# Hash matmuls of two token halves in the two column halves of the array, key bits written with their factor, first load in two parts

## The chip, the cores and the metric

One Trainium2 chip, one of its cores. The metric is the device time of one launch in microseconds (us), the median of the timed runs. The engines are TensorE (PE), VectorE (DVE), ScalarE (ACT), GpSimd (POOL) and the DMA queue fed by SyncE (SP).

## What is computed

Three stages follow each other: hashed attention over 2 x 8 heads, a token and channel mixer, and a mixture of four attention experts. The change is in the first. Cut to what matters there:

```python
q_bits = (np.einsum('bhsd,dk->bhsk', q, proj) > 0)      # 6 bits for each query
k_bits = (np.einsum('bhsd,dk->bhsk', k, proj) > 0)      # 6 bits for each key
mask   = bucket(q_bits)[..., None] == bucket(k_bits)[..., None, :]
scores = np.where(mask, q @ k.T / sqrt(64), -1e9)
attn   = softmax(scores);  out = attn @ v
```

Sequence 768, head dimension 64, 16 heads. Everything is float32 in and out.

## The kernel before

**Tiling.** One head is one turn of the body. Queries come in six tiles of 128 rows, keys in two column halves of 384 (`HALF`). `psS` has two slots of two banks each, in which score tiles and hashes take turns; `psT` takes transposed probabilities, `psO` the products with the values.

**How the mask gets into the scores.** `scores` (L286, L287) adds two products for each key half. Rows 0 to 63 of the operands hold the split parts of queries and keys; rows 64 to 127 of `q_hb` and `k_lb` hold bits. For each of the six bits there is a row for "is one" and a row for "is not one", the key rows multiplied by 2^31 (`BIG`), so that a pair that agrees in all bits gets one common large offset, which the row maximum takes off again.

**The hash.** `hash_both(h+1)` (L259) runs in the body of head h: two fp32 matmuls, one for each token half, with the 128 x 128 projection `pj`, whose blocks give the key hashes on partitions 0 to 37 and the query hashes on 64 to 101. The result fills both banks of the slot that scores(h, 2) needs next. `query_bits` (L464) and `key_bits` (L475) on DVE then read 64 partitions x 768 of it. The query bits go straight to `q_hb`; the key bits go to a bf16 tile `bits`, which POOL multiplies by 2^31 into `k_lb` (`scale_key_bits`, L579).

**Order.** Each engine's order is written out by hand in its `head` function; semaphores join them. On DVE it runs: row_max(h,0) (L440), scale_and_bias (L449, L450), add_halves(h-2,1) (L493), turn(h-1,4) (L457), query_bits(h+1), key_bits(h+1), reciprocals(h-1) (L483, L485), row_max(h,1). On PE: scores(h,0), transposes (L300), hash_both(h+1), value_products(h-1,0) (L317), which waits for add_halves(h-2,1), scores(h,1), transposes, scores(h,2), fold (L328), transposes, scores(h,3), value_products(h-1,1), and so on. scores(h,3) waits for exp(h,1) (L377 on ACT). On POOL: scale_q (L548), round_k (L556), split_k (L563), split_q (L571), scale_key_bits (L579), normalise (L590) twice. ACT's round_q (L402) follows exp(h,0) and releases split_q.

**The start.** A first block builds constants while SP issues the projection and the whole of head 0's q and k (768 KB); a second block issues head 1's and holds the heads. The prologue of head 0 runs on every engine: hash, 12 matmuls on the identity (L63), round and copy q, round k on ACT (L411), split q on POOL, both bit operations and then the k split (L509) on DVE, and L579 on POOL, before scores(0,0).

Of the kernel before, what the change touches and what calls it, by code (L numbers as in the profile page):

```python
# [25 lines left out]
P = 128  # L26
# [6 lines left out]
NB = 6  # L33
NBP = 32 + NB
BIG = 2.0 ** 31
SCALE = 1.0 / D ** 0.5
R = 32
FF = 4 * C
# [75 lines left out]
def hashed_attention(nc, load_mixer, load_mlp_weights, mixer_in, u_rep, qk_2, v_n, proj_2, con, psS, psT, psO, X):  # L114
# [12 lines left out]
    with ExitStack() as ctx:  # L127
# [12 lines left out]
        q8 = sb("q8", [D, S])  # L140
        bits = sb("bits", [P, S], BF16)
        probs = [sb(f"probs{n}", [P, S]) for n in range(3)]
# [7 lines left out]
        rinv = sb("rinv", [P, 2, QT])  # L150
        q_comp = sb("q_comp", [P, 1])
        k_comp = sb("k_comp", [P, 1])
        pj = sb("pj", [P, P])
# [4 lines left out]
        cleared = sem("cleared")  # L158
        hashed = sem("hashed")
        q_bits_made = sem("q_bits_made")  # L160
# [8 lines left out]
        k_split = sem("k_split")  # L169
        kmask_ready = sem("kmask_ready")  # L170
        scores_ready = sem("scores_ready")
# [46 lines left out]
        def start_loads(sp):  # L218
            sp.dma_start(pj[:], proj_2).then_inc(proj_in, 16)
            load_qk(sp, 0, 0)  # L220

        build_constants(nc, ctx, con, start_loads)
        with nc.Block() as block:
            @block.sync
            def _(sp):
                load_qk(sp, 1, 1)
                load_v(sp, 0, 0)

                def next_loads(h, p):
                    sp.wait_ge(kmask_ready, h + 1)  # L230
                    sp.wait_ge(q_copied, h + 1)
                    if not low_bound(h, 1):
# [12 lines left out]
                load_v(sp, LAST - 1, 1)  # L245
                load_mixer(sp)
                load_mlp_weights(sp)

            @block.tensor
            def _(pe):  # L250
                def hash_both(h, p):

                    if not exists(h):
                        return
                    pe.wait_ge(raw_in[p], half_count(h, p))
                    if low_bound(h, 2):
                        pe.wait_ge(exp_done, 6 * (h - 1))
                    for c in range(2):
                        last = nc.tensor.matmul(psS[:, hash_slot(p), c, 0:HALF], pj[:],  # L259
                                                raw[p][:, c * HALF:(c + 1) * HALF], start=True, stop=True)  # L260
                    last.then_inc(hashed, 1)

                def scores(h, p, j):
                    if not exists(h):
                        return
                    slot = score_slot(p, j)
                    if j == 0:
                        pe.wait_ge(kmask_ready, h + 1)
                        pe.wait_ge(q_copied, h + 1)
                        pe.wait_ge(q_bits_made, h + 1)  # L270
                        if low_bound(h, 1):
                            pe.wait_ge(exp_done, 6 * h - 1)
                        else:
                            pe.wait_ge(first_k_split, 1)
                    elif j == 1:
                        pe.wait_ge(exp_done, 6 * h + 1)
                    elif j == 2:
                        if below(h, LAST - 1):
                            pe.wait_ge(q_bits_made, h + 2)
                            pe.wait_ge(k_bits_made, h + 2)  # L280
# [91 lines left out]
            def _(act):  # L372
# [23 lines left out]
                def round_q(h, p):  # L396
                    if not exists(h):
                        return
                    act.wait_ge(raw_in[p], half_count(h, p))
# [9 lines left out]
                def prologue():  # L409
                    round_q(0, 0)  # L410
                    nc.scalar.activation(k_hh[0][:], raw[0][:, S:2 * S], ACT.Copy).then_inc(first_k_rounded, 1)  # L411
                    copy_q(0, 0)

# [21 lines left out]
            def _(dve):  # L435
# [23 lines left out]

                def query_bits(h, p):  # L460
                    if not exists(h):
                        return
                    dve.wait_ge(hashed, h + 1)
                    nc.vector.tensor_scalar(q_hb[p][D:P, :].rearrange("p (c n) -> p c n", c=2),  # L464
                                            psS[D:P, hash_slot(p), :, 0:HALF], 0.0, q_comp[D:P, :],
                                            ALU.is_gt, ALU.subtract).then_inc(q_bits_made, 1)

                def key_bits(h, p):

                    if not exists(h):  # L470
                        return
                    dve.wait_ge(hashed, h + 1)
                    if low_bound(h, 1):
                        dve.wait_ge(kmask_ready, h)
                    nc.vector.tensor_scalar(bits[D:P, :].rearrange("p (c n) -> p c n", c=2),  # L475
                                            psS[0:D, hash_slot(p), :, 0:HALF], 0.0, k_comp[0:D, :],
                                            ALU.is_gt, ALU.subtract).then_inc(k_bits_made, 1)

# [18 lines left out]
                def prologue():  # L497

                    nc.vector.memset(q_comp[:], 0.0)
                    nc.vector.memset(k_comp[:], 0.0).then_inc(cleared, 1)  # L500
                    dve.wait_ge(cleared, 1)
                    nc.vector.memset(q_comp[D + 32:D + 32 + NB, :], 1.0)
                    nc.vector.memset(k_comp[0:NB, :], 1.0).then_inc(cleared, 1)
                    dve.wait_ge(cleared, 2)
# [35 lines left out]
            def _(pool):  # L540

                def scale_q(h, p):
                    if not exists(h):
                        return
                    pool.wait_ge(raw_in[p], half_count(h, p))
                    if low_bound(h, 1):
# [26 lines left out]

                def scale_key_bits(h, p):
                    if not exists(h):
                        return
# [17 lines left out]
                def prologue():  # L594
                    scale_q(0, 0)
                    split_q(0, 0)
                    scale_key_bits(0, 0)

                def head(h, p):
# [3 lines left out]
                    split_q(h + 1, 1 - p)  # L603
                    scale_key_bits(h + 1, 1 - p)
                    normalise(h - 2, p, 1)
# [1067 lines left out]
```

## Time and profile before

| | |
|---|---|
| timed runs, us | 732.81 median of 3 (732.45 to 734.55) |
| the profiled execution's own time, us | 733.43 |
| its span, us | 731.5 |
| busy in the span | PE 694.2 (95%), DVE 384.7 (53%), ACT 390.5 (53%), POOL 298.2 (41%) |
| granted TensorE clock, mean | 0.995 |
| masked heads | from the start to 277 us |

The time outside of the span is 1.9 us. A timeline row gives start, duration, engine, line, operation and tiles (out<-in), the shape, the count merged into the row, and in brackets the idle time of that engine before it with what ended it. Busy shares are averages over three stages; what the change is worth is read from the rows of the first 277 us.

### The profile page before, as it was taken

What the parts mean: (1) busy time and instruction counts of PE and PEld (TensorE: products, weight loads), DVE (VectorE), ACT (ScalarE), POOL (GpSimd) and SP (SyncE); (2) the same over time, 40 slices, a digit from 0 to 9 for tenths busy, and PEclk for the clock granted to TensorE, in tenths of its full rate; (3) what the DMA queues carried; (4) which work ended last, traced back from release to release, by engine and by line L of the source; (5) the groups of instructions that cost most, each with busy time, mean ns of one, the idle gap of its engine ahead of it and who ended that gap; (6) DMA issues with size and microseconds to landing.
All of it is one profiled execution on the core that took longest, in us unless ns stands there. A gap on an engine that the chain in (4) does not pass through costs nothing. (4 is left out here: it accounts for less than half of the span.)

```text
span 731.5 us, 11874 instructions
## 1 busy us (share of the span) xinstructions
PE 694.2 (95%) x3792; PEld 544.9 (74%) x3792; DVE 384.7 (53%) x827; ACT 390.5 (53%) x795; POOL 298.2 (41%) x260
## 2 busy tenths in 40 slices
PE   5899999999999998999999999999999989999986
PEld 3667666667666756788888888888888978788864
DVE  4888888888888846111112111211112757886571
ACT  3777776777777745333333333333333656676662
POOL 6655656545555111444544454345443012331210
PEclk9999999999999999999999999999999999999999
DMA  4112211112210594200000000000000000001102
GB/s 154 44 55 83 80 54 54 54 54 67 93 55 11 102 321 122 58 0 0 0 0 0 0 0 0 0 0 0 0 0 14 17 1 0 2 0 44 44 1 87
DMA packets 27548, 30.58 MB, mean 42 GB/s; under 512 B 11136, under 2 KB 21504, under 8 KB 27520
## 3 DMA queue, kind: packets, MB, share of 16 engines
q1 hardware_dynamic: 27520, 30.23, 13.3%
q8 instruction: 15, 0.25, 0.1%
q14 instruction: 13, 0.11, 0.0%
HBM read 27.07 MB, written 3.15 MB: 41 GB/s over the span
## 5 line engine op out<-in xcount | busy, mean ns | idle before, releaser
L844 DVE SCALAR_TENSOR_TENSOR hid_l<-psT,hid_h 128x512 fp32r<-128x512 f32 x48 | 33.2, 691 | 212.1 <-ACT hid_h L820 212.1
L868 POOL TENSOR_TENSOR w_l<-w_raw,w_h 128x512 fp32r<-128x512 f32 x48 | 62.0, 1293 | 134.6 <-ACT w_h L811 134.6
L377 ACT ACTIVATE probs<-psS,scale_bias 128x768 f32<-128x768 f32 x96 | 95.1, 991 | 37.0 <-DVE scale_bias L450 36.5
L440 DVE TENSOR_REDUCE negmax<-psS 128x1 f32<-128x768 f32 x96 | 91.6, 954 | 9.4 <-PE psS L287 5.2
L300 PE MATMUL psT<-ident,probs 128*128 128x128 f32 x576 | 84.2, 277 | 3.9 <-ACT pt L386 1.8
L300 PEld LDWEIGHTS psT<-ident,probs 128*128 128x128 f32 x576 | 66.3, 140 | 21.5 <-issue 9.6
L811 ACT ACTIVATE w_h<-w_raw 128x512 fp32r (+1 forms) x48 | 30.3, 631 | 95.2 <-PE psS L777 95.2
L286 PE MATMUL psS<-k_hh,q_lh 128*128 128x384 f32 x192 | 73.9, 385 | 5.1 <-ACT probs L377 2.0
L766 PE MATMUL psT<-x_h,w_h 128*128 x192 | 74.9, 390 | 0.7 <-DVEq L836 0.7
L766 PE MATMUL psT<-x_l,w_h 128*128 x192 | 74.9, 390 | 0.0
L766 PE MATMUL psT<-x_h,w_l 128*128 x192 | 74.9, 390 | 0.0
L777 PE MATMUL psS<-hid_h,w_h 128*128 128x512 f32 x192 | 74.8, 390 | 0.0
L777 PE MATMUL psS<-hid_h,w_l 128*128 128x512 f32 x192 | 74.8, 390 | 0.0
L777 PE MATMUL psS<-hid_l,w_h 128*128 128x512 f32 x192 | 74.8, 389 | 0.0
L863 POOL TENSOR_TENSOR w_l<-w_raw,w_h 128x512 fp32r<-128x512 f32 x48 | 62.3, 1298 | 21.2 <-ACT w_h L807 21.2
L317 PE MATMUL psO<-pt,raw_v 128*64 128x384 f32 x384 | 69.0, 495 | 0.0
L820 ACT ACTIVATE hid_h<-psT 128x512 fp32r<-128x512 f32 x48 | 28.8, 600 | 75.3 <-PE psT L766 75.3
L287 PE MATMUL psS<-k_lb,q_hb 128*128 128x384 f32 x192 | 64.7, 337 | 0.0
L457 DVE COPY pt<-psT 128x384 f32<-128x384 f32 x96 | 52.8, 550 | 20.2 <-PE psT L300 20.2
L386 ACT ACTIVATE pt<-psT 128x384 f32<-128x384 f32 x96 | 46.6, 486 | 19.2 <-PE psT L300 19.0
L286 PEld LDWEIGHTS psS<-k_hh,q_lh 128*128 128x128 f32 x192 | 36.2, 189 | 20.2 <-ACT probs L377 9.1
L317 PEld LDWEIGHTS psO<-pt,raw_v 128*64 128x64 f32 x384 | 24.7, 136 | 34.8 <-issue 28.2
(178 smaller groups left out, 1460.1 us busy)
## 6 DMA issues: line engine op xcount, KB each, us to landing
raw<-qk SPq DMA_DIRECT2D x16, 768.0 KB, 4.7
w_raw<-w SPq DMA_DIRECT2D x16, 256.0 KB, 7.1
w_raw<-w SPq DMA_DIRECT2D x4, 1024.0 KB, 8.7
raw_v<-v_n SPq DMA_DIRECT2D x16, 192.0 KB, 2.4
out<-y_out SPq DMA_DIRECT2D x12, 256.0 KB, 2.0
wvg_raw<-wv SPq DMA_DIRECT2D x4, 128.0 KB, 3.5
wqk_raw<-wq SPq DMA_DIRECT2D x4, 128.0 KB, 2.9
wqk_raw<-wk SPq DMA_DIRECT2D x4, 128.0 KB, 3.0
```

Source lines behind the costliest of these rows:

```text
L286: nc.tensor.matmul(psS[:, slot, c, 0:HALF], q_lh[p][:, q], k_hh[p][:, k], start=True, stop=False)
L287: last = nc.tensor.matmul(psS[:, slot, c, 0:HALF], q_hb[p][:, q], k_lb[p][:, k], start=False, stop=True)
L300: last = nc.tensor.transpose(psT[:, c, n * P:(n + 1) * P], probs[j % 3][:, kt * P:(kt + 1) * P], con["ident"][:])
L317: last = nc.tensor.matmul(psO[side * D:(side + 1) * D, c, 0:HALF], raw_v[p][:, kt, :], pt[:, kt, q], start=(kt < 2), stop=(kt >= QT - 2))
L377: nc.scalar.activation(probs[j % 3][:].rearrange("p (c n) -> p c n", c=2), psS[:, score_slot(p, j), :, 0:HALF], ACT.Exp, bias=scale_bias[: ...
L386: nc.scalar.activation(pt[:, 0:TH, j * P:(j + 1) * P], psT[:, 0, 0:HALF].rearrange("p (t q) -> p t q", q=P), ACT.Copy).then_inc(turned[0], 1)
L440: nc.vector.tensor_reduce(negmax[:, p, j:j + 1], psS[:, score_slot(p, j), :, 0:HALF], AXIS.XY, ALU.max, negate=True).then_inc(rowmax_ready, 1)
L457: nc.vector.tensor_copy(pt[:, TH:QT, j * P:(j + 1) * P], psT[:, 1, 0:HALF].rearrange("p (t q) -> p t q", q=P)).then_inc(turned[1], 1)
L766: last = nc.tensor.matmul(psT[:, s, 0:TOK], w[s][:, dt, :], u[:, dt, tok], start=(dt == 0 and m == 0), stop=(dt == DT - 1 and m == 2))
L777: last = nc.tensor.matmul(y[dt], w[s][:, dt, :], h[s][:], start=False, stop=False)
L863: nc.gpsimd.tensor_tensor(w1_l[s][:], w1_raw[:, f, :, :], w1_h[s][:].bitcast(F32), ALU.subtract).then_inc(w1_split, 1)
L868: nc.gpsimd.tensor_tensor(w2_l[s][:].rearrange("p a b -> p (a b)"), w2_raw[:, f, :], w2_h[s][:].rearrange("p a b -> p (a b)").bitcast(F32) ...
```

## The change

- `pj` is 128 x 64 instead of 128 x 128, with one block of the projection for q and one for k; DVE makes the negated blocks at the start.
- Each token half's hash goes to its own 64 partitions of `psS`, both in one bank: half 0 on partitions 0 to 63, half 1 on 64 to 127.
- `bits` on DVE makes query and key bits by four instructions of 32 partitions x 384 each, in place of two of 64 x 768. Both the threshold (`least`) and the factor (`factor`: 1, -1, 2^31, -2^31) are per-partition operands. The key bits go straight into `k_lb`; the bf16 tile and `scale_key_bits` on POOL are gone, and with them the semaphore `kmask_ready`.
- The first load is issued as its q half and its k half; hash, round_q and scale_q of head 0 wait for the first alone.
- The prologue: ACT copies q ahead of rounding k; DVE negates, zeroes four tiles of 32 x 768, sets the two operand columns by small memsets, makes query bits, splits k, makes key bits; PE runs four identity matmuls ahead of the hash.

```diff
+        least = sb("least", [P, 1])
+        factor = sb("factor", [P, 1])
+        pj = sb("pj", [P, D])
...
+            sp.dma_start(raw[0][:, 0:S], qk_2[0, :, 0:S]).then_inc(first_q_in, 16)
+            sp.dma_start(raw[0][:, S:2 * S], qk_2[0, :, S:2 * S]).then_inc(raw_in[0], 16)
...
                 def next_loads(h, p):
-                    sp.wait_ge(kmask_ready, h + 1)
+                    sp.wait_ge(hashed, h + 1)
+                    sp.wait_ge(q_split, h + 1)
                     sp.wait_ge(q_copied, h + 1)
...
-                        last = nc.tensor.matmul(psS[:, hash_slot(p), c, 0:HALF], pj[:],
+                        last = nc.tensor.matmul(psS[c * D:(c + 1) * D, hash_slot(p), 0, 0:HALF], pj[:],
                                                 raw[p][:, c * HALF:(c + 1) * HALF], start=True, stop=True)
...
                     if j == 0:
-                        pe.wait_ge(kmask_ready, h + 1)
+                        pe.wait_ge(q_split, h + 1)
                         pe.wait_ge(q_copied, h + 1)
-                        pe.wait_ge(q_bits_made, h + 1)
+                        pe.wait_ge(q_bits_made, 2 * h + 2)
+                        pe.wait_ge(k_bits_made, 2 * h + 2)
                         if low_bound(h, 1):
+                            pe.wait_ge(k_split, h)
...
                 def prologue():
-                    pe.wait_ge(proj_in, 16)
+                    keep_busy(nc, 4, con, psO[:, 0, :])
+                    pe.wait_ge(negated, 2)
                     hash_both(0, 0)
                     keep_busy(nc, 12, con, psO[:, 0, :])
...
+                def bits(h, p, to, at, made):
+                    if not exists(h):
+                        return
+                    dve.wait_ge(hashed, h + 1)
+                    for c in range(2):
+                        rows = slice(c * D + at, c * D + at + R)
+                        nc.vector.tensor_scalar(to[p][D:D + R, c * HALF:(c + 1) * HALF], psS[rows, hash_slot(p), 0, 0:HALF],
+                                                least[rows, :], factor[rows, :], ALU.is_ge, ALU.mult).then_inc(made, 1)
                 def query_bits(h, p):
...
+                    bits(h, p, q_hb, 0, q_bits_made)
                 def key_bits(h, p):
...
+                    bits(h, p, k_lb, R, k_bits_made)
...
                 def prologue():
...
+                    dve.wait_ge(proj_in, 16)
+                    nc.vector.tensor_scalar(pj[:, NB:2 * NB], pj[:, 0:NB], -1.0, None, ALU.mult).then_inc(negated, 1)
+                    nc.vector.tensor_scalar(pj[:, R:R + NB], pj[:, R + NB:R + 2 * NB], -1.0, None, ALU.mult
+                                            ).then_inc(negated, 1)
...
+                    for p in range(2):
+                        nc.vector.memset(q_hb[p][D + R:P, :].bitcast(F32), 0.0)
+                        nc.vector.memset(k_lb[p][D + R:P, :].bitcast(F32), 0.0)
+                    dve.wait_ge(cleared, 1)
+                    for c in range(2):
+                        nc.vector.memset(least[c * D + R:c * D + R + 2 * NB, :], TINY)
+                        nc.vector.memset(factor[c * D:c * D + 2 * NB, :], -1.0)
+                        nc.vector.memset(factor[c * D + R:c * D + R + 2 * NB, :], BIG).then_inc(cleared, 1)
+                    dve.wait_ge(cleared, 3)
+                    for c in range(2):
+                        nc.vector.memset(least[c * D:c * D + NB, :], TINY)
+                        nc.vector.memset(least[c * D + R:c * D + R + NB, :], 0.0)
+                        nc.vector.memset(factor[c * D:c * D + NB, :], 1.0)
+                        nc.vector.memset(factor[c * D + R:c * D + R + NB, :], -BIG).then_inc(cleared, 1)
+                    dve.wait_ge(cleared, 5)
                     query_bits(0, 0)
-                    key_bits(0, 0)
                     dve.wait_ge(raw_in[0], 16)
                     dve.wait_ge(first_k_rounded, 1)
                     nc.vector.tensor_tensor(k_lb[0][0:D, :], raw[0][0:D, S:2 * S], k_hh[0][0:D, :].bitcast(F32),
                                             ALU.subtract).then_inc(first_k_split, 1)
+                    key_bits(0, 0)
...
-                def scale_key_bits(h, p):
-                    if not exists(h):
-                        return
-                    pool.wait_ge(q_split, h + 1)
-                    pool.wait_ge(k_bits_made, h + 1)
-                    nc.gpsimd.tensor_tensor(k_lb[p][D:P, :], bits[D:P, :], con["big"][D:P, :].to_broadcast([D, S]),
-                                            ALU.mult).then_inc(kmask_ready, 1)
-                    pool.wait_ge(kmask_ready, h + 1)
```

## Rows read from the trace of the kernel before

**Rows 1.** Head loop: stretch, us, busy (count) PE PEld DVE ACT POOL, clock, DMA, GB/s
```profile
100.00:150.00 50.00, 49.17 (x300) 33.84 (x297) 43.16 (x95) 37.11 (x72) 28.06 (x23) 1.00 0.17 59
```

**Rows 2.** Timeline of an odd head, all engines: start us, duration us, engine, line
```profile
138.38 0.96 DVE L440 TENSOR_REDUCE negmax<-psS 128x1 f32<-128x768 f32 x1 [0.21 <-PE psS L287]
...
138.96 1.53 PE L259 MATMUL psS<-raw,pj 128*128 128x384 f32 x4
...
139.57 0.56 DVE L493 TENSOR_REDUCE o_sum<-psO 128x192 f32<-128x384 f32 x1
...
140.42 0.20 PEld L317 LDWEIGHTS psO<-pt,raw_v 128*64 128x64 f32 x4 [0.54 <-DVE o_sum L493]
...
140.63 1.02 DVE L464 TENSOR_SCALAR q_hb<-psS,q_comp 64x768 fp32r<-64x768 f32 x1
...
141.64 1.82 POOL L571 TENSOR_TENSOR q_lh<-q,q_hb 64x768 fp32r<-64x768 f32 x1 [2.08 <-ACT q_hb L402]
141.69 1.01 DVE L475 TENSOR_SCALAR bits<-psS,k_comp 64x768 bf16<-64x768 f32 x1
...
142.73 0.76 DVE L483 TENSOR_SCALAR sums_eps<-sums 128x6 f32<-128x6 f32 x1
...
143.13 0.34 PE L287 MATMUL psS<-k_lb,q_hb 128*128 128x384 f32 x1
...
143.53 1.47 POOL L579 TENSOR_TENSOR k_lb<-bits,big 64x768 fp32r<-64x768 bf16 x1
143.63 0.95 DVE L440 TENSOR_REDUCE negmax<-psS 128x1 f32<-128x768 f32 x1
...
146.06 0.19 PEld L286 LDWEIGHTS psS<-k_hh,q_lh 128*128 128x128 f32 x1 [0.34 <-ACT probs L377]
```

**Rows 3.** Timeline of an even head, the same two steps
```profile
125.71 1.82 POOL L571 TENSOR_TENSOR q_lh<-q,q_hb 64x768 fp32r<-64x768 f32 x1 [1.93 <-ACT q_hb L402]
...
126.84 0.72 DVE L483 TENSOR_SCALAR sums_eps<-sums 128x6 f32<-128x6 f32 x1
```

**Rows 4.** Groups of DVE by form: count, busy us, mean ns of one
```profile
L457 DVE COPY pt<-psT 128x384 f32<-128x384 f32 x96 | 52.8, 550 | 20.2 <-PE psT L300 20.2
...
L450 DVE TENSOR_SCALAR scale_bias<-negmax 128x1 f32<-128x1 f32 x96 | 19.6, 204 | 0.0
...
L449 DVE TENSOR_SCALAR scale_bias<-negmax 128x1 f32<-128x1 f32 x96 | 14.8, 154 | 3.3
...
L951 DVE MEMSET ties<- 128x24 f32 x2 | 0.2, 78 | 0.0
```

**Rows 5.** Timeline of the start and of head 0
```profile
3.03 0.06 DVE L499 MEMSET q_comp<- 128x1 f32 x1 [0.61 <-PEq L79]
...
5.93 0.84 ACT L402 ACTIVATE q_hb<-raw 64x768 fp32r<-64x768 f32 x1 [3.59 <-DMA raw<-qk]
...
6.04 2.90 PE L259 MATMUL psS<-raw,pj 128*128 128x384 f32 x4 [6.04 <-DMA raw<-qk]
...
11.16 0.95 DVE L509 TENSOR_TENSOR k_lb<-raw,k_hh 64x768 fp32r<-64x768 f32 x1
11.27 2.17 POOL L579 TENSOR_TENSOR k_lb<-bits,big 64x768 fp32r<-64x768 bf16 x1 [1.95 <-DVE bits L475]
...
13.49 0.44 PE L286 MATMUL psS<-k_hh,q_lh 128*128 128x384 f32 x1 [1.52 <-POOL k_lb L579]
13.52 1.46 POOL L548 TENSOR_TENSOR q<-raw,eighth 64x768 f32<-64x768 f32 x1
...
16.85 1.01 DVE L475 TENSOR_SCALAR bits<-psS,k_comp 64x768 bf16<-64x768 f32 x1
...
17.93 0.96 DVE L440 TENSOR_REDUCE negmax<-psS 128x1 f32<-128x768 f32 x1
```

**Rows 6.** DMA issues of the run: count, KB each, median us to landing
```profile
raw<-qk SPq DMA_DIRECT2D x16, 768.0 KB, 4.7
...
pj<-proj SPq DMA_DIRECT2D x1, 64.0 KB, 1.8
```

More of the change, by code:

```diff
@@ L36 @@
 SCALE = 1.0 / D ** 0.5
+TINY = 2.0 ** -126
 R = 32
@@ L140, in hashed_attention @@
         q8 = sb("q8", [D, S])
-        bits = sb("bits", [P, S], BF16)
         probs = [sb(f"probs{n}", [P, S]) for n in range(3)]
@@ L158, in hashed_attention @@
         cleared = sem("cleared")
+        negated = sem("negated")
         hashed = sem("hashed")
@@ L169, in hashed_attention @@
         k_split = sem("k_split")
-        kmask_ready = sem("kmask_ready")
         scores_ready = sem("scores_ready")
@@ L219, in start_loads, with wait_q @@
             sp.dma_start(pj[:], proj_2).then_inc(proj_in, 16)
-            load_qk(sp, 0, 0)
+            sp.dma_start(raw[0][:, 0:S], qk_2[0, :, 0:S]).then_inc(first_q_in, 16)
+            sp.dma_start(raw[0][:, S:2 * S], qk_2[0, :, S:2 * S]).then_inc(raw_in[0], 16)
+        def wait_q(eng, h, p):
+            if low_bound(h, 1):
+                eng.wait_ge(raw_in[p], half_count(h, p))
+            else:
+                eng.wait_ge(first_q_in, 16)
         build_constants(nc, ctx, con, start_loads)
@@ L229, in next_loads @@
                 def next_loads(h, p):
-                    sp.wait_ge(kmask_ready, h + 1)
+                    sp.wait_ge(hashed, h + 1)
+                    sp.wait_ge(q_split, h + 1)
                     sp.wait_ge(q_copied, h + 1)
-                    if not low_bound(h, 1):
+                    if low_bound(h, 1):
+                        sp.wait_ge(k_split, h)
+                    else:
                         sp.wait_ge(first_k_split, 1)
@@ L254, in hash_both @@
                         return
-                    pe.wait_ge(raw_in[p], half_count(h, p))
+                    wait_q(pe, h, p)
                     if low_bound(h, 2):
@@ L278, in scores @@
                         if below(h, LAST - 1):
-                            pe.wait_ge(q_bits_made, h + 2)
-                            pe.wait_ge(k_bits_made, h + 2)
+                            pe.wait_ge(q_bits_made, 2 * h + 4)
+                            pe.wait_ge(k_bits_made, 2 * h + 4)
                     else:
@@ L398, in round_q @@
                         return
-                    act.wait_ge(raw_in[p], half_count(h, p))
+                    wait_q(act, h, p)
                     if low_bound(h, 2):
@@ L410, in prologue @@
                     round_q(0, 0)
+                    copy_q(0, 0)
+                    act.wait_ge(raw_in[0], 16)
                     nc.scalar.activation(k_hh[0][:], raw[0][:, S:2 * S], ACT.Copy).then_inc(first_k_rounded, 1)
-                    copy_q(0, 0)
                 def head(h, p):
@@ L463, in query_bits @@
                     dve.wait_ge(hashed, h + 1)
-                    nc.vector.tensor_scalar(q_hb[p][D:P, :].rearrange("p (c n) -> p c n", c=2),
-                                            psS[D:P, hash_slot(p), :, 0:HALF], 0.0, q_comp[D:P, :],
-                                            ALU.is_gt, ALU.subtract).then_inc(q_bits_made, 1)
-                def key_bits(h, p):
-                    if not exists(h):
-                        return
[L472 to L477, printed above, removed]
+                    for c in range(2):
+                        rows = slice(c * D + at, c * D + at + R)
+                        nc.vector.tensor_scalar(to[p][D:D + R, c * HALF:(c + 1) * HALF], psS[rows, hash_slot(p), 0, 0:HALF],
+                                                least[rows, :], factor[rows, :], ALU.is_ge, ALU.mult).then_inc(made, 1)
+                def query_bits(h, p):
+                    bits(h, p, q_hb, 0, q_bits_made)
+                def key_bits(h, p):
+                    bits(h, p, k_lb, R, k_bits_made)
                 def reciprocals(h, p):
@@ L497, in prologue @@
                 def prologue():
-                    nc.vector.memset(q_comp[:], 0.0)
-                    nc.vector.memset(k_comp[:], 0.0).then_inc(cleared, 1)
-                    dve.wait_ge(cleared, 1)
-                    nc.vector.memset(q_comp[D + 32:D + 32 + NB, :], 1.0)
-                    nc.vector.memset(k_comp[0:NB, :], 1.0).then_inc(cleared, 1)
-                    dve.wait_ge(cleared, 2)
+                    dve.wait_ge(proj_in, 16)
+                    nc.vector.tensor_scalar(pj[:, NB:2 * NB], pj[:, 0:NB], -1.0, None, ALU.mult).then_inc(negated, 1)
+                    nc.vector.tensor_scalar(pj[:, R:R + NB], pj[:, R + NB:R + 2 * NB], -1.0, None, ALU.mult
+                                            ).then_inc(negated, 1)
+                    nc.vector.memset(least[:], 0.0)
+                    nc.vector.memset(factor[:], 0.0).then_inc(cleared, 1)
+                    for p in range(2):
+                        nc.vector.memset(q_hb[p][D + R:P, :].bitcast(F32), 0.0)
+                        nc.vector.memset(k_lb[p][D + R:P, :].bitcast(F32), 0.0)
+                    dve.wait_ge(cleared, 1)
+                    for c in range(2):
[9 more added lines that the diff above has]
+                    dve.wait_ge(cleared, 5)
                     query_bits(0, 0)
-                    key_bits(0, 0)
                     dve.wait_ge(raw_in[0], 16)
@@ L544, in scale_q @@
                         return
-                    pool.wait_ge(raw_in[p], half_count(h, p))
+                    wait_q(pool, h, p)
                     if low_bound(h, 1):
@@ L596, in prologue @@
                     split_q(0, 0)
-                    scale_key_bits(0, 0)
                 def head(h, p):
@@ L1654 @@
     qk_2 = np.concatenate([np.concatenate([q_t, k_t], axis=1), np.concatenate([k_t, k_t], axis=1)], axis=2)
-    proj_2 = np.zeros((P, P), np.float32)
-    for at in (0, 32):
-        proj_2[0:D, D + at:D + at + NB] = inputs["proj"]
-        proj_2[D:P, at:at + NB] = inputs["proj"]
+    proj_2 = np.zeros((P, D), np.float32)
+    proj_2[0:D, 0:NB] = inputs["proj"]
+    proj_2[D:P, R + NB:R + 2 * NB] = inputs["proj"]
     laid = {
```

8 lines of the change are left out of this document (1 added, 7 removed).

## The prediction

> **What bounds the kernel now.** I read the busy shares by stretch first. In the head loop PE is busy 49.17 of 50 us and DVE 43.16 [rows 1], so at first sight the 16 hashes on PE are on the path. The timeline of one head says otherwise, and it is to be read backwards from a place where PE waits. scores(h,3) starts at 146.06 after 0.34 us in which PE waited for exp(h,1) [rows 2]. That exponential follows row_max(h,1), which starts on DVE at 143.63 [rows 2]. Two things could have held that row maximum: its scores, and DVE itself. The last score matmul started at 143.13 and took 0.34, so it was over at 143.47 [rows 2]; DVE came free only then: its chain from row_max(h,0) at 138.38 through L493, L464, L475 and L483 has no idle time in it [rows 2]. The last link but one, `sums_eps`, is odd: 128 x 6 elements in 0.76 us, where another small tensor_scalar takes 0.15 to 0.20 [rows 4]. It ends at 142.73 + 0.76 = 143.49, and POOL's split_q (L571) ends at 141.64 + 1.82 = 143.46 [rows 2]. In an even head it is 126.84 + 0.72 = 127.56 against 125.71 + 1.82 = 127.53 [rows 3]. So DVE stands there until POOL's instruction is over. What sets the turn of a head is exp(h,0), round_q on ACT, split_q on POOL, `sums_eps`, row_max(h,1), exp(h,1), scores(h,3), and then PE's own chain to the next scores(h,0). The hash is not in it.
>
> **The hash (PE).** It takes 1.53 us now, four passes [rows 2]; two matmuls side by side should take about half, 0.76. (At the worst nothing is gained, at the best 0.77 a head.) What comes next in PE's order is value_products, which also needs add_halves: that one ends at 139.57 + 0.56 = 140.13, against a start of 140.42 [rows 2]. So PE gets at most 0.3 us of the 0.77, and adds it to its wait of 0.34 ahead of scores(h,3). Value on the path: 0. The Trainium skill's page "TensorEngine Tiling (Array Packing)", section "Performance Considerations", speaks against this edit in the same sense: tiling speeds up TensorE but not the emptying of PSUM. No term of the sum depends on that rule.
>
> **The bit operations (DVE).** Two instructions become four. Now they take 142.73 - 140.63 = 2.10 us from first start to next instruction [rows 2]. The rate along the row, from a 768-wide row maximum (0.96) and a 384-wide copy (0.55), is (0.96 - 0.55)/384 = 1.07 ns an element [rows 2, 4]; half of L464 is then 1.02 - 0.41 = 0.61, and the gap to the next is 141.69 - 140.63 - 1.02 = 0.04 [rows 2], so 0.65 each and 2.60 in all, 0.50 more than now. A second per-partition operand may cost something too: the 128x1 operation with one takes 204 ns, without 154, so 0.05 each bounds it from above, zero from below [rows 4]; four make 2.80. I take zero, since one such operand was already read in L464. The lower end is what two wide ones cost, 2.10, if short ones overlap. What hides the 0.50 is the wait of `sums_eps`: it takes 0.76 and needs at most 0.20, so 0.56 of it are idle [rows 2, 4]. The four end at 140.63 + 2.60 = 143.23, still before split_q's 143.46, and row_max(h,1) stays at 143.63. Value: 0 a head; with the second operand's price they end at 143.43, `sums_eps` at 143.63 instead of 143.49, which makes +0.14 a head. The cover is gone for the first body, where there are no sums: there L475 ends at 16.85 + 1.01 = 17.86 and row_max(0,1) follows at 17.93 [rows 5]. Head 0 pays +0.5, once.
>
> **POOL.** L579 (1.47 us) goes [rows 2], 16 times. It lies behind split_q and ahead of nothing that is awaited: head h+1's scores start some 10 us later. Value 0 in the loop. But normalise now follows split_q directly, as L579 does today, 0.07 behind it (143.53) [rows 2]; if DVE asks for `sums_eps` after that, it stands behind it. The new waits of scores(h,0) and of the loads name work that was over before kmask_ready was; they add nothing, and loads of 4.7 us [rows 6] have a whole head of time.
>
> **The start.** Now: load in at 5.93, hash 6.04 to 8.94, bits, k split at 11.16, L579 11.27 to 13.44, scores(0,0) at 13.49 [rows 5]. After: the half load lands between 64 KB's 1.8 and 768 KB's 4.7 us [rows 6], by a straight line 1.8 + 320/704 x 2.9 = 3.1 us after its issue, which I put at 5.93 - 4.7 = 1.2: 4.3. The hash at the old rate halved takes 1.45: over at 5.8 (bounds 5.8 with the halves side by side, 7.2 one after the other). But DVE isn't ready. From 3.03 [rows 5] it negates twice (0.3), then clears four tiles of 768 columns: a 24-wide clear takes 78 ns, a 1-wide one 60, so 0.8 ns a column, 0.67 each [rows 4, 5]; at 1.07 ns it is 0.88. That is 2.7 to 3.5, I take 2.9. Then 14 small memsets, 0.06 each at least, by twice that at most: 0.8 to 1.7, I take 1.4. Query bits start at 3.03 + 0.3 + 2.9 + 1.4 = 7.6, end at 8.9. Below that, if clears went at twice the rate, 6.2.
> The k split is next. When DVE's k split ran at 11.16, POOL's L579 took 2.17 instead of 1.47 [rows 2, 5]: the two stand in each other's way. In the changed prologue POOL doesn't wait for the bits: it goes on to head 1 (scale_q 1.46 [rows 5], then round_k, split_k) once head 1's load is in, issued at about 3.0, plus 4.7, 7.7. POOL is then busy from 7.7 to 9.2, and again from 9.25. Whichever has begun holds: DVE, ready at 8.9, gets its turn at 9.2, splits until 10.15, makes key bits (1.3) until 11.5, and scores(0,0) starts at 11.6. That is 1.9 earlier. The Trainium skill's page "SBUF — State Buffer", section "Who interferes with whom", has this as a lock: a DVE instruction with two SBUF inputs and a GpSimd instruction that reads SBUF exclude each other for the whole instruction, whoever is first. By it the split waits at POOL's boundary; without it the split would start at 8.9 and the start would gain 2.2.
>
> **The sum.** Start -1.9, head 0 +0.5, the loop 0: -1.4 on the profiled execution's 733.43 = 732.0. That execution is 0.6 above the median of 732.81, so 731.4 on the median's scale.
>
> **Rivals.**
> 1. *DVE misses POOL's boundary.* Ready after 9.2 (clears at 0.88, or small memsets at 0.12), the split waits for round_k's end at 10.7; scores(0,0) at 13.1. Start -0.4, with head 0 +0.1: 732.9. For: only 0.3 us separate the two. Chance 0.15.
> 2. *The start opens fully.* Clears at twice the rate or smaller memset costs; DVE is at the split before 7.7: it runs 7.7 to 8.65, scores(0,0) at 10.1, -3.4 + 0.5: 729.9. Against: the 24-wide clear's 0.8 ns. Chance 0.14.
> 3. *PE is the bound after all.* The hash's 0.77 counts in 15 heads (head 0's is in the start): -11.6 - 1.4: 719.8. For: PE busy 98% [rows 1]. Against: the 0.34 wait, and 140.13 against 140.42. Chance 0.07.
> 4. *The second operand costs 0.05.* +0.14 in 14 heads, +2.0, and head 0 +0.2: 733.6. Chance 0.14.
> 5. *Slower: the cliff at `sums_eps`.* If an operation takes more than (143.53 - 140.63)/4 = 0.725 from start to start, DVE comes when POOL has begun normalise (some 0.5 of POOL) and stands behind it. row_max(h,1) then slips by about 0.6 in each of 14 heads: +8.4 - 1.4: 739.8. My 0.65 leaves 0.075; the second operand would eat 0.05 of it. Chance 0.10.
> 6. *The halves don't run side by side.* Hash as long as now: nothing changes in the loop, at the start the hash ends at 7.2, still before DVE's 7.6: 731.4 again. It has no chance of its own.
>
> The forecast holds 0.38; the last 0.02 is for what I haven't seen.
>
> **How the numbers follow.** The measurement tells 0.3% (2.2 us) from no change. Faster is below 730.6: rivals 2 and 3 (0.21) and a quarter of the forecast (0.10), 0.31. Slower is above 735.0: rival 5 (0.10) and tails of rivals 4 and 1, 0.17. The same: 0.52. The range leaves out rivals 3 and 5 (0.17) and so runs from 728.5, a little under rival 2, to 736.0, rival 4 with head 0's surplus doubled.
>
> **What would show it.** The distance from split_q of an even head to that of the next (141.64 - 125.71 = 15.93 now [rows 2, 3]) should stay within 0.05; the first score matmul should start at 11.6 instead of 13.49; the bit instructions should start 0.65 apart; `sums_eps` should shrink to some 0.2 to 0.3 and still end just behind split_q; PE's idle time ahead of scores(h,3) should grow from 0.34. I am wrong in the loop if the period falls by 0.3 or more (the hash was on the path) or grows by 0.5 (the cliff), and at the start if the k split does not wait for POOL, or DVE is ready before 7 or after 9.2.

## The result: 1.1% slower

| | before | after |
|---|---|---|
| median of the timed runs, us | 733.68 (4 runs, 732.45 to 734.66) | 740.65 (4 runs, 740.17 to 743.63) |
| span of the profiled execution, us | 731.5 | 738.5 |
| granted clock, mean | 0.995 | 0.991 |

The ratio after to before is 1.0113, 95% interval 1.0087 to 1.0138 (an estimate of its own; the quotient of the two medians is 1.0095). The medians are 7.0 us apart, where I had forecast 731.4 within 728.5 to 736.0, which was 1.4 us under the 732.81 that stood there for the kernel before. The value that came is that of rival 5 (739.8), to which I had given 0.10.

The page of the changed kernel, span and busy times of the engines:

```profile
span 738.5 us, 11934 instructions
...
PE 690.4 (93%) x3800; PEld 543.1 (74%) x3800; DVE 396.9 (54%) x877; ACT 391.3 (53%) x795; POOL 274.3 (37%) x244
```

PE and POOL do less than before and DVE does 12 us more. The same stretch of the head loop as in [rows 1] (stretch, length, busy us and count of PE, PEld, DVE, ACT, POOL, clock, DMA share, GB/s):

```profile
100.00:150.00 50.00, 45.88 (x286) 31.75 (x286) 43.90 (x97) 35.44 (x69) 22.57 (x18) 1.00 0.17 59
```

PE has come down from 49.17 to 45.88 busy us: in part by the shorter hash, in part because these 50 us now hold 3.05 heads instead of 3.16. It now waits more than before. The odd head that answers to [rows 2], timeline:

```profile
141.70 0.96 DVE L456 TENSOR_REDUCE negmax<-psS 128x1 f32<-128x768 f32 x1 [0.32 <-PE psS L301]
...
142.24 0.87 PE L271 MATMUL psS<-raw,pj 128*64 128x384 f32 x4
...
142.94 2.10 PE L331 MATMUL psO<-pt,raw_v 128*64 128x384 f32 x12
...
143.94 1.38 DVE L483 TENSOR_SCALAR q_hb<-psS,least,factor 32x384 fp32r<-32x384 f32 x2
...
144.95 1.81 POOL L599 TENSOR_TENSOR q_lh<-q,q_hb 64x768 fp32r<-64x768 f32 x1 [2.17 <-ACT q_hb L417]
...
145.35 1.39 DVE L483 TENSOR_SCALAR k_lb<-psS,least,factor 32x384 fp32r<-32x384 f32 x2
...
146.73 0.50 POOL L609 TENSOR_TENSOR X<-o_sum,rinv 128x192 f32 x1
146.77 0.49 DVE L496 TENSOR_SCALAR sums_eps<-sums 128x6 f32<-128x6 f32 x1
...
147.52 0.96 DVE L456 TENSOR_REDUCE negmax<-psS 128x1 f32<-128x768 f32 x1
...
149.95 0.19 PEld L300 LDWEIGHTS psS<-k_hh,q_lh 128*128 128x128 f32 x1 [0.34 <-ACT probs L392]
```

Read it against [rows 2]. The hash (L271) takes 0.87 instead of 1.53 us, and value_products (L331) start 142.94 - 141.70 = 1.24 after row_max(h,0) instead of 140.42 - 138.38 = 2.04. So PE's edit worked, in full. From row_max(h,0) to row_max(h,1), though, it is now 147.52 - 141.70 = 5.82 us instead of 143.63 - 138.38 = 5.25. The four bit operations take 146.77 - 143.94 = 2.83, 0.71 each. `sums_eps` (L496) is issued at 146.77; POOL's normalise (L609) had begun at 146.73, at the very end of split_q (L599, 144.95 + 1.81 = 146.76). `sums_eps` then ends at 147.26, 0.03 after normalise: it is recorded as 0.49 us long, and takes 0.16 where POOL is idle (e1 below). scores(h,3), at 149.95, wait 0.34 for exp(h,1) as before; the time that PE has gained it now waits for DVE ahead of them, in the transposes (L314) that need the copy (L473) which DVE makes after row_max(h,1). The view of waits, 100 to 250 us (who waited for whom: us in total, times, longest), had no row of PE's matmuls before:

```profile
PE psT L314 <- DVE pt L473: 8.3, 10, 0.8
PE psS L300 <- DVE k_lb L483: 1.3, 5, 0.3
```

An even head, against [rows 3]:

```profile
128.38 1.83 POOL L599 TENSOR_TENSOR q_lh<-q,q_hb 64x768 fp32r<-64x768 f32 x1 [1.93 <-ACT q_hb L417]
...
130.17 0.50 POOL L609 TENSOR_TENSOR X<-o_sum,rinv 128x192 f32 x1
130.19 0.51 DVE L496 TENSOR_SCALAR sums_eps<-sums 128x6 f32<-128x6 f32 x1
```

Here normalise began 0.02 us ahead of `sums_eps`, and held it again. The profile's round_q positions give the length of a head over the 13 periods from the third to the sixteenth: before 29.78 to 235.45, 15.82 us; after 29.52 to 242.28, 16.37 us. 13 x 0.55 = 7.1.

The start, against [rows 5]:

```profile
4.44 0.84 ACT L417 ACTIVATE q_hb<-raw 64x768 fp32r<-64x768 f32 x1 [2.10 <-DMA raw<-qk]
...
4.97 1.55 PE L271 MATMUL psS<-raw,pj 128*64 128x384 f32 x4
...
8.04 1.38 DVE L483 TENSOR_SCALAR q_hb<-psS,least,factor 32x384 fp32r<-32x384 f32 x2
9.45 0.95 DVE L536 TENSOR_TENSOR k_lb<-raw,k_hh 64x768 fp32r<-64x768 f32 x1
9.53 2.19 POOL L576 TENSOR_TENSOR q<-raw,eighth 64x768 f32<-64x768 f32 x1 [1.70 <-DMA raw<-qk]
...
12.09 0.41 PE L300 MATMUL psS<-k_hh,q_lh 128*128 128x384 f32 x1 [2.56 <-DVE k_lb L483]
...
15.77 1.39 DVE L483 TENSOR_SCALAR k_lb<-psS,least,factor 32x384 fp32r<-32x384 f32 x2
...
17.19 0.96 DVE L456 TENSOR_REDUCE negmax<-psS 128x1 f32<-128x768 f32 x1
```

The first scores come at 12.09 instead of 13.49, 1.4 earlier. Head 0 gives most of it back: by the third round_q (29.52 against 29.78) 0.26 is left, so 1.14 are lost. Two things are in that. The bits delay row_max(0,1) (15.77 + 1.39 = 17.16, then 17.19; 4.13 after row_max(0,0) instead of 3.44). And PE's granted clock falls to half, 1.2 GHz: it is 0.90 over 12 to 14 us, 0.50 from 14 to 20 and 0.90 over 20 to 22. PE had sat idle from 9.5 to 12.1 before that, and again from 13.9 to 15.5. Its matmuls of 384 columns take 0.52 instead of 0.34 us, and row_max(0,2) waits for them:

```profile
14.00:16.00 2.00, 0.51 (x2) 0.51 (x3) 1.86 (x6) 1.64 (x3) 1.02 (x1) 0.50 0.15 56
16.00:18.00 2.00, 1.84 (x6) 1.36 (x5) 1.94 (x3) 0.17 (x1) 1.69 (x1) 0.50 0.00 0
18.00:20.00 2.00, 2.00 (x10) 1.90 (x9) 1.43 (x5) 1.48 (x3) 1.57 (x2) 0.50 0.00 0
```

```profile
18.96 0.96 DVE L456 TENSOR_REDUCE negmax<-psS 128x1 f32<-128x768 f32 x1 [0.51 <-PE psS L301]
```

In the kernel before the clock is 1.00 over the first 30 us. So: start and head 0 -0.3, heads +7.1, in all +6.8; the spans differ by 7.0.

### The profile page after: what moved, and what is told of

The parts are those of the page before. It is cut to its first block and busy times, and to the rows that moved or that the text cites. A ratio compares the mean times of both kernels' runs of the same rounds, so it can differ in the third digit from the quotient of the medians.

```text
span 738.5 us, 11934 instructions
## 1 busy us (share of the span) xinstructions
PE 690.4 (93%) x3800; PEld 543.1 (74%) x3800; DVE 396.9 (54%) x877; ACT 391.3 (53%) x795; POOL 274.3 (37%) x244
## 3 DMA queue, kind: packets, MB, share of 16 engines
HBM read 27.04 MB, written 3.15 MB: 41 GB/s over the span
## 5 line engine op out<-in xcount | busy, mean ns | idle before, releaser
L314 PE MATMUL psT<-ident,probs 128*128 128x128 f32 x576 | 86.8, 278 | 15.2 <-DVE pt L473 11.4
L314 PEld LDWEIGHTS psT<-ident,probs 128*128 128x128 f32 x576 | 66.9, 141 | 34.9 <-DVE pt L473 20.7
L331 PE MATMUL psO<-pt,raw_v 128*64 128x384 f32 x384 | 68.5, 491 | 0.0
L473 DVE COPY pt<-psT 128x384 f32<-128x384 f32 x96 | 52.8, 550 | 20.2 <-PE psT L314 20.2
L609 POOL TENSOR_TENSOR X<-o_sum,rinv 128x192 f32 (+1 forms) x32 | 16.2, 505 | 106.4 <-DVE o_sum L506 106.4
```

The costliest lines, as they stand in the source:

```text
L314: last = nc.tensor.transpose(psT[:, c, n * P:(n + 1) * P], probs[j % 3][:, kt * P:(kt + 1) * P], con["ident"][:])
L331: last = nc.tensor.matmul(psO[side * D:(side + 1) * D, c, 0:HALF], raw_v[p][:, kt, :], pt[:, kt, q], start=(kt < 2), stop=(kt >= QT - 2))
L473: nc.vector.tensor_copy(pt[:, TH:QT, j * P:(j + 1) * P], psT[:, 1, 0:HALF].rearrange("p (t q) -> p t q", q=P)).then_inc(turned[1], 1)
```

## The experiments

Each table value is a median, with the ratio to the kernel before in the same session. "Period" is the length of a head from its profile, by round_q positions. The two kernels of the case: 15.82 and 16.37. Times of the kernel before were 732.1, 732.0 and 733.0 in the three sessions (733.7 in the first comparison), so the ratios are what is to be compared.

| run | us | ratio (95%) | period |
|---|---|---|---|
| changed kernel | 740.65 | 1.0113 (1.0087 to 1.0138) | 16.37 |
| e1_recip_first | 735.2 | 1.0044 (1.0027 to 1.0062) | 15.91 |
| e2_normalise_first | 735.99 | 1.0049 (1.0028 to 1.0071) | 16.07 |
| e3_immediate | 733.91 | 1.0028 (1.0007 to 1.0048) | 15.94 |
| e4_hash_twice | 739.61 | 1.0103 (1.0081 to 1.0125) | 16.39 |
| e5_short_early | 730.02 | 0.9971 (0.9955 to 0.9986) | 15.67 |
| e6_before_recip_first | 731.73 | 0.9996 (0.9979 to 1.0012) | 15.78 |
| e7_bits_late | 742.71 | 1.0139 (1.0118 to 1.0161) | 16.67 |
| e8_keep_busy | 738.75 | 1.0084 (1.0058 to 1.0109) | 16.38 |
| e9_hold_pool | 729.35 | 0.9952 (0.9937 to 0.9966) | 15.67 |
| e10_bits_placed | 726.7 | 0.9912 (0.9897 to 0.9927) | 15.37 |

**e1: reciprocals ahead of the bits.** My theory: what costs is `sums_eps` behind normalise. The rival: the four operations are longer than the two, and that is all.

```diff
+                    reciprocals(h - 1, 1 - p)
                     query_bits(h + 1, 1 - p)
                     key_bits(h + 1, 1 - p)
-                    reciprocals(h - 1, 1 - p)
```

> The changed kernel with reciprocals(h-1) ahead of the two bit operations on DVE, nothing else. Theory (DVE stands behind POOL's normalise at sums_eps): sums_eps then runs while POOL is idle, in 0.16 us; the bits follow 0.3 later and row_max(h,1) starts 3.16 after the turn instead of 3.58: 0.42 less in each of 13 heads, so about 5.5 us under the changed kernel's 740.65, 735.2. Rival (only the length of the four bit operations counts): no change, 740.6. Rival (PE's wait for the key bits counts): slower, the bits end 0.3 later, 744.

It came as the theory had it: the same instructions in another order give 0.46 a head back. In its trace `sums_eps` takes 0.16 us:

```profile
141.71 0.16 DVE L496 TENSOR_SCALAR sums_eps<-sums 128x6 f32<-128x6 f32 x1
```

**e2: the same from POOL's side.** DVE's order stays; POOL does its normalise where it would wait for ACT.

```diff
-                    split_q(h + 1, 1 - p)
                     normalise(h - 2, p, 1)
+                    split_q(h + 1, 1 - p)
```

> The changed kernel with POOL's normalise(h-2, 1) ahead of split_q, in the 2 us in which POOL waits for round_q. DVE's order stays. Theory: sums_eps finds POOL free when it comes, 0.01 behind split_q's end; it takes 0.16 instead of 0.5, row_max(h,1) comes 0.34 earlier, 13 heads, 4.4 us: 736.2. Rival (length of the bit operations alone): 740.6.

The timeline shows the order changed and the wait gone:

```profile
142.81 0.51 POOL L609 TENSOR_TENSOR X<-o_sum,rinv 128x192 f32 x1 [0.82 <-DVE o_sum L506]
...
144.12 1.83 POOL L599 TENSOR_TENSOR q_lh<-q,q_hb 64x768 fp32r<-64x768 f32 x1 [0.80 <-ACT q_hb L417]
...
145.94 0.17 DVE L496 TENSOR_SCALAR sums_eps<-sums 128x6 f32<-128x6 f32 x1
```

`sums_eps` takes 0.17 although it comes just as split_q ends. 0.30 a head, 0.34 forecast; the median too is within 0.2 us of it, though the seven times of this run spread from 733.73 to 739.96.

**e3: 0.05 us less in each bit operation.**

```diff
-                                                least[rows, :], factor[rows, :], ALU.is_ge, ALU.mult).then_inc(made, 1)
+                                                0.0, factor[rows, :], ALU.is_gt, ALU.mult).then_inc(made, 1)
```

> The changed kernel with the threshold of the bit operations as the constant 0 (greater than) instead of the per-partition operand; it differs only where a hash is exactly zero or denormal. Theory: one operand less takes 0.05 off each of four operations, 0.68 to 0.63; the bits then end before split_q does, DVE is in the queue ahead of normalise, and row_max(h,1) comes 0.55 to 0.6 earlier, not 0.2: 13 heads, 7.5 us: 733.1. Rival (cost in proportion to the length): 0.2 a head, 738.0. Rival (the second operand costs nothing): 740.6.

This is the sharpest of them: the four operations are shorter by 2.83 - (143.41 - 140.82) = 0.24 us together, and the head by 0.43, since DVE now stands in the queue before POOL gets to normalise:

```profile
140.82 1.26 DVE L483 TENSOR_SCALAR q_hb<-psS,factor 32x384 fp32r<-32x384 f32 x2
...
141.84 1.82 POOL L599 TENSOR_TENSOR q_lh<-q,q_hb 64x768 fp32r<-64x768 f32 x1 [2.14 <-ACT q_hb L417]
...
143.41 0.28 DVE L496 TENSOR_SCALAR sums_eps<-sums 128x6 f32<-128x6 f32 x1
...
143.62 0.50 POOL L609 TENSOR_TENSOR X<-o_sum,rinv 128x192 f32 x1
```

Per operation that is 0.65 from start to start instead of 0.71. The four end at 143.38, `sums_eps` ends at 143.69, just behind split_q (143.66), and normalise, begun at 143.62, doesn't hold it. The forecast time was 733.1; 733.9 came, the period fell 0.43 instead of 0.57. In proportion to the work it would have been 0.24.

**e4: hash twice.** Is PE's part on the path in the changed kernel?

```diff
-                    for c in range(2):
+                    for c in (0, 1, 0, 1):
```

> The changed kernel with each hash matmul issued twice, so that PE spends on it what it did before the change. Theory (the hash is not on the path): the first bit operation is ready at 0.1 us either side of the hash's end, so 740.6 to 742. Rival (PE bound): 0.73 in 15 heads, 751.

```profile
145.10 1.51 PE L271 MATMUL psS<-raw,pj 128*64 128x384 f32 x8
...
146.81 1.38 DVE L483 TENSOR_SCALAR q_hb<-psS,least,factor 32x384 fp32r<-32x384 f32 x2
```

PE spends twice as long and the period moves by 0.02. So in the loop the saving on PE is worth nothing in this order of the work. The period is what shows it; the median (739.61) can't weigh the start. In this run's profile the third round_q comes at 32.12, 2.6 later than in the changed kernel, and a stretch of half clock that the changed kernel's profile has later on (0.59 over 594 to 598 us) is absent here (1.00).

**e5: both mendings.** The constant threshold of e3 and the order of e1.

```diff
-                                                least[rows, :], factor[rows, :], ALU.is_ge, ALU.mult).then_inc(made, 1)
+                                                0.0, factor[rows, :], ALU.is_gt, ALU.mult).then_inc(made, 1)
...
+                    reciprocals(h - 1, 1 - p)
                     query_bits(h + 1, 1 - p)
                     key_bits(h + 1, 1 - p)
-                    reciprocals(h - 1, 1 - p)
```

> The changed kernel with both mendings: the constant threshold (0.63 instead of 0.68 an operation) and reciprocals ahead of the bits. Theory: DVE's chain from row_max(h,0) to row_max(h,1) is then 5.38 - 4 x 0.06 = 5.13 us, against 5.27 in the kernel before; nothing of POOL is in it. 13 heads x 0.14 = 1.8 under the kernel before, and the start adds -0.2: 2.0 under the kernel before. Rival (PE is next and holds the period): the same time as the kernel before within 0.5.

2.0 us forecast, 2.0 measured, period 15.67 against 15.68.

```profile
136.55 0.96 DVE L456 TENSOR_REDUCE negmax<-psS 128x1 f32<-128x768 f32 x1 [0.32 <-PE psS L301]
...
140.45 0.34 PE L301 MATMUL psS<-k_lb,q_hb 128*128 128x384 f32 x1
...
141.69 0.96 DVE L456 TENSOR_REDUCE negmax<-psS 128x1 f32<-128x768 f32 x1
```

row_max(h,1) comes 5.14 after row_max(h,0); its scores were over at 140.79, so DVE's own chain holds it. With POOL out of DVE's chain the change turns from a loss into a small gain (ratio 0.9971, interval below 1).

**e6: the mending alone, on the kernel before.**

```diff
+                    reciprocals(h - 1, 1 - p)
                     query_bits(h + 1, 1 - p)
                     key_bits(h + 1, 1 - p)
-                    reciprocals(h - 1, 1 - p)
```

> The kernel before with reciprocals ahead of its two bit operations. Theory: DVE's chain is shorter by the 0.56 wait for POOL, but scores(h,1) end only 0.12 (odd heads) or 0 (even heads) ahead of today's row_max(h,1), so the gain is 0.06 a head: 1 us or less. Rival (the POOL wait was the only bound): 0.5 a head, 7 us.

```profile
138.18 0.96 DVE L440 TENSOR_REDUCE negmax<-psS 128x1 f32<-128x768 f32 x1 [0.20 <-PE psS L287]
...
143.32 0.96 DVE L440 TENSOR_REDUCE negmax<-psS 128x1 f32<-128x768 f32 x1 [0.53 <-PE psS L287]
```

No difference that the measurement can tell, as the theory wanted: with POOL out of the way row_max(h,1) waits 0.53 for PE's scores(h,1). It also means that the 0.56 us wait of the kernel before was cover, not cost. That the faster hash is what lets e5 pass e6 is argued, not shown: the intervals of the two ratios overlap, and no run has e5's order with the slow hash. The profiles leave it little: in e4, with the doubled hash, scores(h,1) are over 4.9 (odd heads) to 5.1 us (even heads) after row_max(h,0), still ahead of e5's 5.13.

**e7: bits made late, from SBUF.** If DVE's chain to row_max(h,1) is the bound, the bits should leave it. ACT copies the hashes out of PSUM, DVE makes the bits from SBUF later, with e3's constant threshold.

```diff
+                def copy_hashes(h, p):
...
+                    nc.scalar.activation(hashes[:], psS[:, hash_slot(p), 0, 0:HALF], ACT.Copy).then_inc(hash_copied, 1)
...
-                    query_bits(h + 1, 1 - p)
-                    key_bits(h + 1, 1 - p)
                     reciprocals(h - 1, 1 - p)
...
                     add_halves(h - 1, 1 - p, 0)
+                    late_bits(h + 1, 1 - p, q_hb, 0, q_bits_made)
+                    late_bits(h + 1, 1 - p, k_lb, R, k_bits_made)
```

> Constant threshold; ACT copies both hash halves to SBUF right after exp(h,0) (0.49 us), which frees the PSUM slot, and DVE makes the four bit tiles from SBUF after add_halves(h-1,0), where it waits 1.1 us for PE. Theory: row_max(h,1) is then held by PE alone, and here the shorter hash counts, since add_halves no longer hides more than half of it: 0.35 a head, less what 1.7 us of bits do beyond the 1.1 us of cover: 1 to 4 us under the kernel before. Rival (the bits merely move the delay to turn(h,1)): 2 us over the kernel before.

A miss: 10.7 us over the kernel before, where I forecast 1 to 4 under it and the rival was 2 over; and by the mechanism that I had just shown. The timeline has both halves of it:

```profile
136.82 0.99 DVE L503 TENSOR_SCALAR q_hb<-hashes,factor 32x384 fp32r<-32x384 f32 x2
...
137.56 1.57 POOL L596 TENSOR_TENSOR q<-raw,eighth 64x768 f32<-64x768 f32 x1
...
137.84 1.96 DVE L503 TENSOR_SCALAR k_lb<-hashes,factor 32x384 fp32r<-32x384 f32 x2
...
139.83 0.56 DVE L483 COPY pt<-psT 128x384 f32<-128x384 f32 x1
...
144.03 0.96 DVE L466 TENSOR_REDUCE negmax<-psS 128x1 f32<-128x768 f32 x1 [0.36 <-PE psS L302]
...
148.31 0.96 DVE L466 TENSOR_REDUCE negmax<-psS 128x1 f32<-128x768 f32 x1 [1.77 <-PE psS L302]
```

row_max(h,1) does come 4.28 after row_max(h,0), 0.97 sooner than in the kernel before. But from SBUF a pair of bit operations takes 0.85 only where POOL is idle (e10 below); here the second pair meets POOL's scale_q (137.56 to 139.13) and takes 1.96, and turn(h,1) (L483, 139.83), for which PE waits, comes about 2 us late. So the rival was right in kind: the delay moved to turn(h,1).

**e8: PE kept busy at the start.** More identity matmuls between hash and first scores.

```diff
                     hash_both(0, 0)
-                    keep_busy(nc, 12, con, psO[:, 0, :])
+                    keep_busy(nc, 22, con, psO[:, 0, :])
```

> The changed kernel with 22 instead of 12 identity matmuls between hash and first scores. In the changed kernel PE idles 2.6 us there and its granted clock is 0.50 from 16 to 20 us. Theory: the clock stays at 1.0 in head 0 and about 0.7 us come back: 740.0. Rival (head 0 is held by DVE, not by PE's clock): the clock stays up and the time is unchanged. If the clock falls all the same, what PE did before the scores doesn't decide it.

The ratio's interval overlaps that of the changed kernel, so no gain is shown. In its profile the clock is at 0.95 from 16 to 18 and at 0.50 from 18 to 24 us: the fall comes later, not never, so what PE did before the scores doesn't decide it alone. What a kept clock would be worth this run can't say. And the profile shows something better, the start's other wait:

```profile
9.26 1.46 POOL L576 TENSOR_TENSOR q<-raw,eighth 64x768 f32<-64x768 f32 x1 [1.50 <-DMA raw<-qk]
9.45 2.12 DVE L536 TENSOR_TENSOR k_lb<-raw,k_hh 64x768 fp32r<-64x768 f32 x1
```

The key split took 2.12 us, because POOL's scale_q had begun 0.19 before it (9.26 + 1.46 = 10.72, and then its own 0.9), and the first scores came at 13.29. In the changed kernel's own profile above it was DVE that came first, 0.08 ahead, and POOL took 2.19.

**e9: POOL held at the start.** e5 and one line.

```diff
                     split_q(0, 0)
+                    pool.wait_ge(first_k_split, 1)
```

> Run e5 with POOL's work for head 1 held until DVE has split head 0's keys. Theory: that split then always takes 0.95 us, never up to 2.1 as in the profiles in which POOL's scale_q had begun first, and the first scores start at 11.9 to 12.1 in every execution: up to 1.1 us under e5's 730.0 in some executions, 0.5 on the median: 729.5. Rival (head 1 misses what POOL now does later): 730.5.

```profile
9.34 0.95 DVE L536 TENSOR_TENSOR k_lb<-raw,k_hh 64x768 fp32r<-64x768 f32 x1
```

729.35, and its split takes 0.95. The ratio went from 0.9971 to 0.9952 with overlapping intervals: in the forecast direction, not shown by the times alone.

**e10: e7's bits where POOL is idle.** With e9's hold.

```diff
                     turn(h, p, 0)
+                    late_bits(h + 1, 1 - p, q_hb, 0, q_bits_made)
                     row_max(h, p, 3)
                     scale_and_bias(h, p, 3)
+                    late_bits(h + 1, 1 - p, k_lb, R, k_bits_made)
```

> Run e7 with its late bit operations put where POOL is idle: the query bits after turn(h,0), the key bits after scale_and_bias(h,3), and with e9's hold. In e7 row_max(h,1) came 4.28 us after row_max(h,0) (5.25 in the kernel before), but one bit operation stood 1.2 us behind POOL's scale_q and turn(h,1) came 2 us late. Theory: without that wait the bits cost 0.4 each, 1.6 in all, some 1.1 of it in the time in which DVE waits for PE; the period falls from 15.68 (e5) to about 15.3: 725. Rival (row_max(h,3), later by 0.8, holds exp(h,3) and scores(h,5)): period 15.9 or more, 733.

```profile
135.55 0.96 DVE L466 TENSOR_REDUCE negmax<-psS 128x1 f32<-128x768 f32 x1 [0.31 <-PE psS L302]
...
139.84 0.96 DVE L466 TENSOR_REDUCE negmax<-psS 128x1 f32<-128x768 f32 x1 [1.77 <-PE psS L302]
...
143.24 0.85 DVE L503 TENSOR_SCALAR q_hb<-hashes,factor 32x384 fp32r<-32x384 f32 x2
...
145.43 0.86 DVE L503 TENSOR_SCALAR k_lb<-hashes,factor 32x384 fp32r<-32x384 f32 x2
```

The same bit operations as in e7, at two other places of DVE's order: one pair in head 0 takes 1.33 us, all later ones 0.85 or 0.86, never 1.96, and the interval from row_max(h,0) to row_max(h,1) stays at 4.29 (4.45 in even heads). The period is 15.37 (15.3 forecast), the time 726.7 (725 forecast). It beats both kernels, by 0.9% the kernel before, and its interval lies below those of e5 and e9 too. Rival 2 of its expectation (exp(h,3) held) has not come.

## Why the prediction was wrong, step by step

- **What bounds the loop: right for the changed kernel, half right for the one before.** The chain through DVE, with `sums_eps` ending just behind a POOL instruction, is what the experiments moved. e4 shows that the hash isn't on it, e1 and e2 that the POOL wait is. But in the kernel before I had called the POOL wait what sets the turn of a head, and e6 took it away for 0.04 us a head: PE's scores(h,1), behind the slow hash and value_products, were over only 0.04 us ahead of row_max(h,1) in even heads and 0.16 in odd ones (143.47 against 143.63).
- **The hash, value 0: right in value, wrong in one of its two reasons.** Side by side it took 0.87 (I had 0.76). But I wrote, in the prediction and in the description of the kernel, that value_products wait for add_halves(h-2,1), and that PE would keep at most 0.3. In the changed kernel they start at 142.94, before that add_halves (from 142.89, 0.56 long) is over. By the count in their `wait_ge(sum_done, 2 * h - 1 + c)` they wait for the other half's, add_halves(h-2,0), of long before; the "[0.54 <-DVE o_sum L493]" of [rows 2] was no wait, the weight load stood behind the running hash. PE keeps 0.8 us a head and gives it back waiting for DVE. That e10's interval from row maximum to row maximum, in which DVE waits 1.77 for PE, is 0.96 shorter than in the kernel before (4.29 against 5.25) shows what PE can do with the short hash.
- **The bit operations, value 0: wrong. This is the step that failed**, by its size first. I put 0.65 from start to start and "I take zero" for the second per-partition operand; it was 0.71. e3 isolates the operand: 0.62 against 0.68 an operation, and with one operand they start 0.65 apart, as I had put it. So the term that I put at nothing is what was missing: 4 x 0.06 = 0.24 us a head, and with it 0.21 more of waiting for POOL (`sums_eps` takes 0.49 for e3's 0.28). e3 gives back 0.43 by taking it out. What is left of e3, 0.12 a head over the kernel before, I can't account for: there row_max(h,1) starts 0.25 after `sums_eps` has ended (143.69, 143.94), before it was 0.14 (143.49, 143.63). The bound of 0.05 that I had worked out from [rows 4] was close to the truth, and I took the other end.
- **The edge, at 0.725 in rival 5: wrong too.** I took it from L579, which starts 0.07 behind split_q [rows 2]. But L579 waits for a semaphore of split_q and normalise waits for nothing: it starts 0.03 ahead of split_q's recorded end. The edge was at (146.73 - 143.94)/4 = 0.70. With 0.71 even the right operand price would have seemed safe against 0.725. Taking L579 away moved the edge, and this I had written down as "value 0 in the loop".
- **Rival 5: right in mechanism and size.** +0.57 from row maximum to row maximum against my 0.6. That its sum fits so well is in part luck: I took 14 heads at 0.6 (+8.4) where the 13 periods gave +7.1, and -1.4 for the start and head 0 where -0.3 came, so +7.0 stands beside +6.8 although neither term fits as well. Rival 4, the same operand price without the edge, is what I had thought more likely.
- **The start: -1.9 forecast, -1.4 came, and not by the path I gave.** Clears took 0.70 each (I had 0.67 to 0.88) but started 0.8 apart, 3.15 in all for my 2.9; what stands ahead of them took 0.49 for my 0.3; the 14 small ones took the 1.4 that I gave them. DVE was ready at 8.04 instead of 7.6. The two side by side hash matmuls took 1.55 (1.45). I had POOL begin at 7.7 and the key split wait for it. Head 1's load let POOL begin at 8.1 or later, and not twice at the same time, so who comes first at the key split is a matter of chance. In the changed kernel's own profile the split (9.45) was first and did not wait, which I had named as a sign of being wrong. Over the eight profiles without e9's hold it took 0.95 in three, 1.08 in one (POOL first and soon over, as in the forecast) and 1.66 to 2.12 in four (POOL first and late, with the first scores at 12.8 to 13.3, close to rival 1's 13.1).
- **Head 0: +0.5 forecast, about +1.1 came.** The bits gave 0.7 of it (4.13 against 3.44). The rest I hadn't seen. The half clock from 14 to 20 us is there in the profile, and so is row_max(0,2)'s wait of 0.51 for the slowed matmuls; that nothing else is in the rest is argued, not shown, since e8 did not keep the clock up.

On the lock, the Trainium skill's page "SBUF — State Buffer", section "Who interferes with whom", agrees with what came. By it a DVE instruction in a two-port mode, or one with two SBUF inputs beside a POOL instruction that reads SBUF, and the POOL instruction exclude each other, and the second to come waits until the first is over; a DVE instruction with at most one SBUF input, outside those modes, doesn't take part. The bit operations reading PSUM were never held (1.38 to 1.40 a pair with POOL busy beside them), those reading SBUF were (0.85 a pair with POOL idle, 1.96 behind scale_q).

## What to carry to other kernels

A wait can be cover for work that is added ahead of it, but look at what its engine does next: here being 0.04 us late cost some 0.4 us a head (e3), since the instruction behind the one waited for took another half microsecond. When a step is taken off an engine, ask what now moves up into its place and whom that meets. And an instruction that must not meet another engine's is best put where that engine is idle: e10, with the bit operations there, is 0.9% under the kernel before, and e9, with them in DVE's chain to row_max(h,1), 0.5%.

## What I hadn't expected of the hardware

- A second per-partition operand costs 0.06 us in a 32 x 384 tensor_scalar from PSUM (0.68 against 0.62). The two 128x1 ones of L449 and L450, 0.05 apart, differ by one such operand and by one arithmetic step besides.
- Clears of 32 x 768 that take 0.70 us start 0.80 apart (3.50, 4.30, 5.11, 5.92).
- The load of head 1 (768 KB behind the two half loads) lands at different times from one profile to the next: POOL, waiting for it, starts at 8.09, 8.79, 8.96, 9.12 or 9.26 in five profiles, and at 9.53 to 10.35 in three more.
- TensorE's granted clock fell to half (1.2 GHz) by 14 us and stayed there to 20, although PE had matmuls again from 12.1 to 13.9 us; it had been idle from 9.5 to 12.1 and was idle again to 15.5. In the kernel before PE was idle from 12.0 to 13.5 and from 15.7 to 16.9, and the clock stayed at 1.00.
